# Attention by pairs of heads: half-height scores, V held on half the columns, and denominators from the exponential

## The reference

```python
# attention, 4 batches x 12 heads x 448 positions x 64; g_q and g_k are gains of 64
def rmsnorm(x, g):
    rms = np.sqrt(np.mean(x * x, axis=-1, keepdims=True) + 1e-06)
    return x / rms * g
q_n, k_n = (rmsnorm(q, g_q), rmsnorm(k, g_k))
scores = 1.0 / np.sqrt(64) * np.matmul(q_n, k_n.transpose(0, 1, 3, 2))
scores = scores - np.max(scores, axis=-1, keepdims=True)
attn = np.exp(scores)
attn = attn / (np.sum(attn, axis=-1, keepdims=True) + 1e-09)
x = np.matmul(attn, v)            # then heads side by side: 1792 tokens x 768
# experts: 8 experts, 768 -> 1024 -> 768
logits = (x / (|x| + 1e-06)) @ (emb / (|emb| + 1e-06)).T / tau
expert = argmax(logits); gate = softmax(logits)[expert]
y = gate * (relu(x @ w1[expert]) @ w2[expert])
# gated layer, 768 -> 1536 -> 768
out = (sigmoid(y @ w_gate) * (y @ w_val)) @ w_out
```

## Time and profile before

| | |
|---|---|
| median of 3 runs | 1302.7 us (1301.39 to 1303.6) |
| span of the profiled execution | 1302.7 us |
| attention, from the start to routing's first reduction | 386.4 us |
| PE busy | 1218.3 us (94%), 8578 records |
| PEld busy | 1152.2 us (88%) |
| DVE busy | 724.4 us (56%) |
| ACT busy | 617.2 us (47%) |
| POOL busy | 252.7 us (19%) |

### The profile page before, as it was taken

One profiled execution on the slowest core, in us unless ns is written; L12 is line 12 of the kernel. 1 busy time (PEld: TensorE's weight loads), 2 busy tenths in 40 slices (PEclk: granted clock), 3 DMA queues, 4 the chain that ended last, 5 costly groups with the idle time before them and its releaser, 6 DMA issues. The chain is left out here.

```text
span 1302.7 us, 25062 instructions
## 1 busy us (share of the span) xinstructions
PE 1218.3 (94%) x8578; PEld 1152.2 (88%) x8579; DVE 724.4 (56%) x1376; ACT 617.2 (47%) x1151; POOL 252.7 (19%) x265
## 2 busy tenths in 40 slices
PE   6999999999980799989999899999999999999996
PEld 5999999999970799989999899999999999999995
DVE  5888888888874465546656633333342343333432
ACT  5777777777640455445555533323332333233321
POOL 5565565565534000000000000001000100010001
PEclk9999999999985799989999999999999999999998
DMA  2112111111115977648877553334334434344332
GB/s 75 44 43 53 42 42 50 45 42 43 32 29 177 226 204 189 151 128 214 221 189 185 156 147 114 104 98 149 111 100 116 140 97 121 97 139 117 100 101 62
DMA packets 259960, 146.33 MB, mean 112 GB/s; under 512 B 30914, under 2 KB 255170, under 8 KB 259854
## 3 DMA queue, kind: packets, MB, share of 16 engines
q1 hardware_dynamic: 257367, 134.86, 38.6%
q0 software_dynamic: 2560, 11.02, 2.6%
HBM read 133.94 MB, written 11.92 MB: 112 GB/s over the span
## 5 line engine op out<-in xcount | busy, mean ns | idle before, releaser
L1228 POOL DMA_INDIRECT out_dram<-rows,idp x16 | 18.1, 1133 | 866.4 <-DVE rows L1190 862.7
L558 PE MATMUL av<-V,PT 112*112 112x65 f32 x1536 | 175.2, 257 | 0.0
L558 PEld LDWEIGHTS av<-V,PT 112*112 112x112 f32 x1536 | 166.1, 178 | 0.3 <-DVE PT L350 0.2
L1181 DVE TENSOR_TENSOR gv<-vb,sg 128x448 f32<-128x448 f32 x48 | 30.0, 625 | 218.1 <-PE vb L1246 218.1
L343 DVE TENSOR_REDUCE negmax<-sc 112x1 f32<-112x448 f32 x192 | 118.9, 619 | 57.4 <-PE sc L531 57.3
L452 ACT ACTIVATE PR<-sc,negmax 112x448 f32<-112x448 f32 x192 | 121.9, 635 | 35.2 <-DVE negmax L343 34.0
L1022 PE MATMUL hb<-XH,W1H 128*128 128x256 f32 (+1 forms) x384 | 112.1, 292 | 11.0 <-issue 6.5
L1022 PE MATMUL yb<-HH,W2H 128*128 128x256 f32 (+1 forms) x384 | 112.7, 293 | 0.0
L1137 ACT ACTIVATE l_WH<-stream 128x768 fp32r<-128x768 f32 x100 | 82.3, 840 | 62.6 <-PE vb L1246 60.8
L1023 PE MATMUL hb<-XL,W1H 128*128 128x256 f32 (+1 forms) x384 | 111.4, 290 | 0.0
L1024 PE MATMUL hb<-XH,W1L 128*128 128x256 f32 (+1 forms) x384 | 111.4, 290 | 0.0
(11 more groups left out here) (179 smaller groups left out, 2933.3 us busy)
## 6 DMA issues: line engine op xcount, KB each, us to landing
raw<-in_moe_w_dram SPq DMA_DIRECT2D x66, 384.0 KB, 5.2
stream<-in_moe_w_dram SPq DMA_DIRECT2D x48, 512.0 KB, 4.6
stream<-in_moe_w_gate_dram SPq DMA_DIRECT2D x34, 384.0 KB, 3.5
stream<-in_moe_w_val_dram SPq DMA_DIRECT2D x34, 384.0 KB, 4.0
stream<-in_moe_w_out_dram SPq DMA_DIRECT2D x32, 384.0 KB, 3.8
xr<-x_sorted SPq DMA_DIRECT2D x9, 768.0 KB
l_raw<-in_moe_w_gate_dram SPq DMA_DIRECT2D x16, 384.0 KB, 3.4
l_raw<-in_moe_w_val_dram SPq DMA_DIRECT2D x16, 384.0 KB, 4.0
```

The costliest lines, as they stand in the source:

```text
L558: last = nc.tensor.matmul(av[n % 2][0:P, j * (D + 1):(j + 1) * (D + 1)], PT[:, j, i * P:(i + 1) * P], V[:, s, i, :], start=(i == 0), stop= ...
L1181: nc.vector.tensor_tensor(gv[:, f % 2, :], vb[f % 2][:, 0:S], sg[:, f % 2, :], ALU.mult).then_inc(prod, 1)
```

## The change

Everything in attention is done for two heads at a time, 24 pairs.

- The turned q and k have head 0 on partitions 0 to 63 and head 1 on 64 to 127 (one turn serves both heads), each as a high and a low part over all partitions: QH, QL, KH, KL, two slots each.
- A block of scores is three products for each head (QH x KH, QH x KL, QL x KH), each on 64 partitions, issued alternately for the two heads, into two banks. The two `sc` tiles take four banks; one maximum covers both heads.
- The exponential also gives the sum of its row (`accum_out`), which is the denominator. V has no column of ones.
- `tpa` and `tpb` (one bank each) take the turned probabilities of head 0 and head 1; ACT copies head 0's four blocks and head 1's even ones, DVE head 1's odd ones.
- `mix` holds V (64 columns) and moves PT over all 448 positions; head 0 writes partitions 0 to 63 of `av` and head 1 64 to 127. It is called four times for a pair, with two products in each. The output is already turned: ACT copies it to oT, `route` reads that, and `turn_rows` turns it back into `tpb`, from where DVE multiplies with the reciprocals straight into X. The logits are scaled by the reciprocals as they are copied, 16 columns for a pair.
- POOL squares q and k; `raw` and V have two slots of a pair. SP loads with half as many DMAs of twice the size, with `load_v` ahead of `load_qk` in each step.
- LP has a row for each head instead of each pair.

```diff
+        raw = sb("raw", [P, 2, 2, 2, NT * D])
...
+        KH = sb("KH", [128, 2, S], F32R)
+        KL = sb("KL", [128, 2, S], F32R)
+        V = sb("V", [P, 2, 2, NT, D])
+        negmax = sb("negmax", [P, 2, NT, 2])
+        PR = sb("PR", [P, 2, NT, S])
+        PT = sb("PT", [P, 2, 2, NT, S])
+        den = sb("den", [P, 2, 2, NT])
+        rden = sb("rden", [P, 2, 2, NT])
+        oT = sb("xT", [128, S])
...
+        sc = [ps(f"sc{i}", [128, 2, 512]) for i in range(2)]
+        tpa = ps("tpa", [128, 512])
+        tpb = ps("tpb", [128, 512])
+        av = ps("av", [128, 512])
...
+            def load_v(it, n):
+
+                if there(it, n):
+                    p, s = 2 * it + n, n % 2
+                    if there(it, n - 2):
+                        sp.wait_ge(mixed, p - 1)
+                    sp.dma_start(V[:, s, :, :, :].rearrange("p h t d -> p h (t d)"),
+                                 v_h[heads_of(it, n), :, :].rearrange("h p x -> p h x")).then_inc(v_in[s], 16)
...
+                load_v(it, n + 1)
+                load_qk(it, n + 4)
...
+            def squares(it, n):
+
+                if there(it, n):
+                    p, s = 2 * it + n, n % 2
+                    pool.wait_ge(qk_in[s], 32 * rounds(it, n))
+                    if there(it, n - 2):
+                        pool.wait_ge(summed, 2 * p - 2)
+                    for i in range(2):
+                        x = raw[:, s, i, :, :].rearrange("p h x -> p (h x)")
+                        nc.gpsimd.tensor_tensor(sq[:, s, i, :], x, x, ALU.mult).then_inc(squared, 1)
...
+            def step(it, n):
+                squares(it, n + 3)
+                x_squares(it, n - 3)
+                over_rms(it, n + 2)
...
+                    nc.vector.tensor_reduce(negmax[:, n % 2, j, :], sc[j % 2][0:P, :, 0:S], AX.X, ALU.max,
                                            negate=True).then_inc(maxed, 1)
...
+            def x_rows(it, n):
+
+                if there(it, n):
+                    p, s = 2 * it + n, n % 2
+                    dve.wait_ge(row_turned, p + 1)
+                    dve.wait_ge(den_step, 2 * p + 2)
+                    r = rden[:, s, :, :].rearrange("p h t -> p t h").unsqueeze(3).to_broadcast([P, NT, 2, D])
+                    nc.vector.tensor_tensor(c.X[:, :, heads_of(it, n), :],
+                                            tpb[0:P, :].rearrange("p (t h d) -> p t h d", h=2, d=D), r,
+                                            ALU.mult).then_inc(x_ready, 1)
...
+            def low(it, n, i, LO, HI, done, hi_done):
+
+                if there(it, n):
+                    p, s = 2 * it + n, n % 2
+                    dve.wait_ge(hi_done, p + 1)
+                    nc.vector.scalar_tensor_tensor(out=LO[:, s, :], in0=tqk[:, 0:S], scalar=gains[:, i:i + 1],
+                                                   in1=HI[:, s, :].bitcast(F32), op0=ALU.mult,
+                                                   op1=ALU.subtract).then_inc(done, 1)
...
+                x_rows(it, n - 3)
+                row_max(it, n, 0)
+                logits(it, n - 3)
+                pair_squares(it, n - 4)
+                row_max(it, n, 1)
+                b_copy(it, n - 1, 3)
+                sums(it, n + 2, 0)
+                row_max(it, n, 2)
+                low(it, n + 1, 0, QL, QH, q_lo, q_hi)
+                sums(it, n + 2, 1)
+                over_den(it, n - 1)
                 row_max(it, n, 3)
+                low(it, n + 1, 1, KL, KH, k_lo, k_hi)
+                b_copy(it, n, 1)
...
+                    for h in range(2):
+                        nc.scalar.activation(PR[:, h, j, :], sc[j % 2][0:P, h, 0:S], ACT.Exp,
+                                             bias=negmax[:, s, j, h:h + 1],
+                                             accum_out=den[:, s, h, j:j + 1]).then_inc(exped, 1)
...
+                a_copy(it, n - 1, 2)
+                b_copy(it, n - 1, 2)
                 exp(it, n, 0)
+                a_copy(it, n - 1, 3)
                 exp(it, n, 1)
+                out_T(it, n - 2)
+                a_copy(it, n, 0)
+                b_copy(it, n, 0)
+                high(it, n + 1, 0, QH, q_hi, q_turned)
                 exp(it, n, 2)
+                a_copy(it, n, 1)
+                high(it, n + 1, 1, KH, k_hi, k_turned)
                 exp(it, n, 3)
...
+                for i, (QX, KX) in enumerate(((QH, KH), (QH, KL), (QL, KH))):
+                    for h in range(2):
+                        rows = slice(h * D, (h + 1) * D)
+                        last = nc.tensor.matmul(sc[j % 2][0:P, h, 0:S], QX[rows, s, cols], KX[rows, s, :],
+                                                start=(i == 0), stop=(i == 2))
+                last.then_inc(scored, 1)
...
+                for h in range(2):
+                    last = nc.tensor.matmul(av[h * D:(h + 1) * D, 0:S], V[:, s, h, i, :],
+                                            PT[:, s, h, :, i * P:(i + 1) * P], start=(i == 0), stop=(i == NT - 1))
+                if i == NT - 1:
                     last.then_inc(mixed, 1)
...
+                pe.wait_ge(oT_out, p + 1)
+                if there(it, n + 2):
+                    pe.wait_ge(b_out_dve, 2 * p + 5)
+                else:
+                    pe.wait_ge(b_out_dve, 2 * PAIRS)
+                    if there(it, n - 1) and not there(it, n + 1):
+                        pe.wait_ge(x_ready, p)
+                for t in range(NT):
+                    last = nc.tensor.transpose(tpb[0:P, t * 128:(t + 1) * 128], oT[:, t * P:(t + 1) * P], c.ident[:, :])
+                last.then_inc(row_turned, 1)
...
+                scores(it, n, 0)
+                turn_probs(it, n - 1, 2)
+                mix(it, n - 2, 2)
+                route(it, n - 3)
+                scores(it, n, 1)
+                turn_probs(it, n - 1, 3)
+                mix(it, n - 2, 3)
+                turn(it, n + 1, 0)
+                scores(it, n, 2)
+                turn_probs(it, n, 0)
+                mix(it, n - 1, 0)
+                turn(it, n + 1, 1)
+                scores(it, n, 3)
+                turn_probs(it, n, 1)
+                mix(it, n - 1, 1)
+                turn_rows(it, n - 2)
+            pipeline(step, -1, PAIRS + 2, pe, {0: turn_emb})
```

More of the change, by code:

```diff
@@ L220, in pipeline @@
                     after[n]()
-            with eng.Fori(1, 11) as it:
-                for n in range(4):
+            with eng.Fori(2, 10) as it:
+                for n in range(2):
                     step(it, n)
-            for n in range(44, last + 1):
+            for n in range(20, last + 1):
                 step(0, n)
@@ new lines, in b_copy, with high @@
+            def b_copy(it, n, j):
+                if there(it, n):
+                    act.wait_ge(b_turned, 4 * (2 * it + n) + j + 1)
+                    nc.scalar.activation(PT[:, n % 2, 1, j, :], tpb[0:P, 0:S], ACT.Copy).then_inc(b_out_act, 1)
+            def high(it, n, i, HI, done, turned):
+                if there(it, n):
+                    act.wait_ge(turned, 2 * it + n + 1)
+                    nc.scalar.activation(HI[:, n % 2, :], tqk[:, 0:S], ACT.Copy, scale=gains[:, i:i + 1]).then_inc(done, 1)
@@ L545, in turn_probs @@
-                last.then_inc(turned, 1)
-            def mix(it, n, j):
+                    last = nc.tensor.transpose(tpa[0:P, cols], PR[:, 0, j, cols], c.ident[0:P, 0:P])
+                last.then_inc(a_turned, 1)
+                pe.wait_ge(exped, 8 * p + 2 * j + 2)
+                if j % 2:
+                    pe.wait_ge(b_out_act, 2 * p + j // 2 + 1)
+                elif j or there(it, n - 1):
+                    pe.wait_ge(b_out_dve, 2 * p + j // 2)
+                if j == 2 and there(it, n - 2):
+                    pe.wait_ge(x_ready, p - 1)
@@ new lines, in route @@
+            def route(it, n):
+                if not there(it, n):
+                    return
+                p = 2 * it + n
+                if not there(it, n - 1):
+                    pe.wait_ge(enT_ready, 2)
+                if there(it, n + 3):
+                    pe.wait_ge(k_lo, p + 4)
+                if there(it, n - 1):
+                    pe.wait_ge(routed_out, p)
+                for t in range(NT):
+                    out = tqk[0:P, S + t * 2 * E:S + (t + 1) * 2 * E]
+                    last = nc.tensor.matmul(out, oT[:, t * P:(t + 1) * P],
+                                            enT[:, bass.ds(p, 1), :, :].rearrange("p a h e -> p (a h e)"),
+                                            start=True, stop=True)
+                last.then_inc(routed, 1)
```

423 lines of the change are left out of this document (163 added, 260 removed).

## The result

The changed kernel takes 1317.5 us (median of four runs, 1312.9 to 1320.4) against 1302.05 of the kernel before, run beside it on the same chip: a ratio of 1.0114, 95% interval 1.0091 to 1.0137. It is slower by 1.1%, 15 us. The forecast was 1340 us, slower by 37. The sign was right and the size was off by more than half.

What follows compares the result with a forecast made beforehand. PE was taken to set attention's pace: 15.2 us of own work plus 1.3 of waits, 16.6 a pair; 19.2 + 24 x 16.6 + 9 = 426.6 against 386.4, so 1302.7 + 37 = 1340 us, range 1315 to 1362.

Steps and rivals of the forecast that it cites:

- the mix call: PE's mix of two heads: records partly side by side, three times 0.37, 1.12 us a call, 4.5 a pair.
- the change of shape: PE switching between full and half array: 0.19 us each (bounds 0 to 0.23), 16 a pair, 3.0 us.
- the fourth: Rival: mix side by side also from call to call, 0.75 us; pair 15.9, kernel 1323 us; no separate chance given.
- the forecast's own walk: One pair through PE and the queues: turn q at 0, turn k 4.3, rows 8.7, next turn q 16.6 us.
- the third step: Rows to next turn of q: inputs in time, no waits, 8 changes of shape; from 8.7 to 16.6 us.
- an end taken too short: After the pairs (out_T, rows, route, logits): as long as today's, 9 us in the sum.
- the credit for first and last steps: Start and end of attention: 2 us taken off because those steps miss a part of the waits.
- scores side by side: PE's score products: two heads' half-row products run together, 0.69 us a block, 2.8 a pair.
- PE idle before turn k for QL and before the rows for PT of b: PE waits on ScalarE's and VectorE's queues at these two places, 1.3 us a pair together.
- The first: Rival: halves side by side, shape changes cost next to nothing; 1278 us, or 1295 at 0.05 a change; chance 0.25.
- The second and third: Rivals, halves not side by side: without shape changes 1351 us, chance 0.09; with changes paid 1412 us, chance 0.09.
- The sixth: Rival: near no change in kernel time, from a shape change at 0.08 us; chance 0.05.

Runs made afterwards that it cites:

- probe: Changed kernel with head 1 moving half its columns in mix calls 1 to 3 (work left out); pair 15.29 us against 15.30.
- onecol: Changed kernel with both heads' products on the same 64 columns in mix calls 1 to 3 (work left out); pair 16.79 us against 15.30.
- byhead: Changed kernel with a block's six score products issued head by head instead of alternating; 1314.2 us (a single run), pair 15.33 us.
- padhole: Changed kernel with each pair's first mix call, ahead of the wait for QL, made twice; 1319.1 us, pair 15.29 us.
- padroute: Changed kernel with each pair's routing products made twice, in the stretch without a wait; 1333.6 us, pair 16.07 us.
- start: On top of "both": pair 0's squares on ScalarE, earlier sums, its multiplication on VectorE, pair 1's normalization ahead of pair 2's squares on GpSimd; 1265.3 us (0.9710).
- both: Changed kernel with mixes two and two ahead of PE's waits, and high and low parts earlier in ScalarE's and VectorE's queues; 1268.8 us (0.9745).
- onerow: Changed kernel with all six score products of a block on the same 64 rows (work left out); pair 17.7 us at full clock against 15.30.
- highfirst: Changed kernel with high and low parts moved ahead in ScalarE's and VectorE's queues, PE's order untouched; 1292.4 us (0.9927), pair 14.42 us.
- mixfull: Changed kernel with V held over all 128 columns and only head 0's PT moved in the mix (work left out); pair 14.70 us against 15.30.

## Why the prediction was right in its sign and wrong in its size

**The failed step is the mix call.** The forecast said: "Head 0's second must follow its first, head 1's first may run beside head 0's second, head 1's second follows: three times 0.37, 1.12 us". Both heads run beside each other in both records, 0.75 us of streams in a call and 0.90 with the change of shape (probe, onecol); with 0.75 in its place PE's own work is 1.5 us a pair less than forecast. It was listed as a rival (the fourth), but its case for it, calls that overlap one another, was not the reason. The step that led there was "in order", taken for a fact although no row of the trace showed it. In probe head 1's second record even starts ahead of head 0's second (207.6 and 207.8), and byhead shows for the scores that the order of issue doesn't decide.

**The second mis-sized term is the change of shape,** 0.19 where 0.12 to 0.15 was measured. It was read off one place with 8 rows; the direction and the count of sixteen were right.

**Why this came to 1.3 us a pair and not 2.1.** Four calls at 0.37 and sixteen changes at 0.04 would make the pair 2.1 us shorter. But the forecast's own walk says where it counts. From turn q to turn k it had 4.3 us, from there to the rows 4.4, set by ScalarE's and VectorE's queues; measured (the rows of the pair above, with the turn of Q at 211.08 and the next of K at 215.31) are 4.23 and 4.33. Both steps stand within 0.1 although the mixes inside them were overpriced, since cheaper mixes only lengthen the waits: 0.6 and 0.7 forecast, 1.03 and 1.12 found. Only the third step, from the rows to the turn of Q, was wrong: 7.9 forecast, 15.30 - 8.56 = 6.74 found (6.81 in the pair shown, 204.27 to 211.08). It holds two mixes (0.75 too much) and eight changes (0.05 each for the rest). padhole and padroute show just this: a mix is free in the one place, and work counts whole in the other. The sign, too, comes from there. PE's own work alone (13.15 us) would have made the kernel faster; that the slower side was right rests on the walk through the queues, whose first two steps held.

**The rest of the sum.** Pairs: 24 x 1.3 = 31 us less than forecast. Start: 19.57 for 19.2, as forecast. The end and the first pairs: 402.50 - 19.57 - 24 x 15.30 = 15.7 where 9 less 2 was taken, 9 us more. The same sum for the kernel before is 386.36 - 13.27 - 24 x 15.12 = 10.2. So 1.2 of the 9 is an end taken too short, 2 are the credit for first and last steps, which did not show, and 5.5 are new. (A small slip lies beside it: 40.2 less 2 is 38, not 37.)

Most of the 5.5 is a wait of VectorE that the forecast named nowhere. DVE and PE in order of time:

```profile
25.89 0.20 DVE L433 TENSOR_SCALAR en<-en,tau_sb 8x1 f32<-8x1 f32 x1 [6.46 <-POOL en L327]
...
29.35 0.71 PE L559 MATMUL sc<-KH,QH 64*112 64x448 f32 x2 [2.92 <-ACT PR L469]
```

Pair 0's first scores have ended by about 21.1 us, but VectorE has the scaling of the embedding ahead of their maximum, and for that it waits 6.5 us for GpSimd, which comes to the embedding only behind pair 1's normalization. The maximum starts at 26.85 and the third block of scores at 29.35; the 3.3 us that pair 1's transposes stood (25.41) ran beside this. In "start", with GpSimd's order changed, the maximum starts at 21.12, and from the first score to the first turn of the rows it takes 35.6 us (18.48 to 54.11) instead of 40.3 in "both" (19.59 to 59.90), 4.7 less. TensorE's clock rises earlier there as well (between 29 and 31 us, in "both" near 35), so this wait and the slower clock are not told apart in the 4.7. At the end, routing's reduction waits 1.86 us, 0.32 in the earlier trace rows: PE's last records end by 397.9, but GpSimd's last power of attention runs from 399.88 for 2.27 us, so it probably waits for that, which no run tested. The two together are enough for the 5.5. So 22 us too much: 37 forecast, 15 found.

**Right as forecast:** scores side by side at 0.69 a block (onerow: 1.3 without); PE idle before turn k for QL and before the rows for PT of b; clock full; first score; ScalarE's 9.8 us a pair (37.71 x 15.3 / 60 = 9.6); GpSimd's power of 16 elements at 2.9 (2.93 in the rows of "start"). VectorE's maximum, at most 1.24, took 1.09 (201.38 in the rows of "highfirst").

**The rivals.** The first (changes near nothing, 1278) had PE's gain right in kind and the cause wrong: the changes do cost. The second and third fall with onecol and onerow, whose lengthened calls and blocks are what they would have looked like. The fourth (1323) was nearest to the time. The sixth, near no change, is out too (1.0091 to 1.0137). The first rival's time is reached, but by another way: the change's gain of 2 us on PE's own work was there all along, held up by two waits that its order of work had made. With the holes filled it comes out, and the kernel is 2.1% faster than before; with both edits and the start, 2.9%.

## What to carry to other kernels

Before pricing an engine's work, cut its loop at its waits and ask of each piece who sets its length. Only in the pieces that this engine sets does every price of its own count. In the others, what stands behind the work that the other engines wait for turns into idle time or out of it, and what stands ahead of that work still counts; a gain on the busiest engine comes out when its work is moved into the waits. When a conversion is moved ahead in a queue, look at what it overtook and who waits behind that. And a price that hangs on "in order" needs a row that shows the order to matter.

## What was not expected of the hardware

- Products on different row or column halves don't keep to the order of issue: in byhead the program has head 0's three products first, and the records still come as three couples (203.36, 203.65, 203.85); in probe head 1's short second record starts at 207.6, ahead of head 0's second at 207.8. Only a spread of three products was tried.
- A half-array product costs per record what a full one does (0.37 us for 448 fp32 columns: a mix call of two full-width records in mixfull, 0.76, streams as long as one of four half-width ones), so the halves give two for one in streams, and a change of shape around them takes 0.12 to 0.15 us.
- An exponential with its sum out brings a second instruction of 0.21 us behind it on ScalarE; in the changed kernel one exponential starts 0.61 us after the other (28.58 and 29.19), where one without the sum has the next instruction 0.53 behind it. Group from 60 to 340 us:

```profile
L469 ACT ACTIVATION_READ_ACCUMULATOR PR<-sc,negmax 112x1 f32 x146 | 31.1, 213 | 0.0
```

- In "onerow" the granted clock fell to its lower level (1.2 GHz) in pieces of attention, with PE listed busy for 4.00 of 4.00 us, and pairs there took 22.6 us and more. Before the fall at 180.4 us the engine ran its ordinary order of scores, transposes and mixes, and before the rise at 190.5 it did the same. The columns below are those of the stretch above. Two other runs have one short fall each in the last outputs of attention: "start" (337.2 to 340.4) and "padroute" (405 to 408). In "start" PE had stood 0.87 us for ScalarE just before, in "padroute" it had run transposes and the doubled routing products. In the others it falls only when PE's work of attention has ended, or, in the kernel before, just ahead of its last eight records. Why it fell in these three was not settled.

```profile
184.00:188.00 4.00, 4.00 (x15) 3.10 (x15) 1.62 (x3) 0.00 (x0) 0.00 (x0) 0.50 0.00 0
```

- The clock column reads 1.00 from the start of a run, and the digit line of the earlier trace rows a 9, but the lengths say otherwise. In the changed kernel four transposes take 0.99 us before 43 us and 0.60 behind, and 0.99 is what the same group takes in "onerow" at a granted clock of 0.50 (187.10). So the lower level holds until about 43.5 us, in the kernel before until about 22 (a second score product of 0.57 us at 20.08, of 0.36 at 22.34). Before it rose, PE had run scores and transposes since 39.6 with no wait for another engine named.

```profile
41.00 0.99 PE L573 MATMUL tpa<-ident,PR 112*112 112x112 f32 x4
43.87 0.60 PE L573 MATMUL tpa<-ident,PR 112*112 112x112 f32 x4
```
